# Two fused feed-forward layers: token tiles of 512 columns in place of 480

## The chip, the cores and the metric

One core of one Trainium2 chip. The time is device microseconds of one execution of the program; the median of several runs counts, lower is better.

## What is computed

```python
# x, v: (1, 12480, 128); pos_emb: (12480, 64)
h_filt = (relu(pos_emb @ w1) @ w2) * exp(-0.01 * pos)[:, None]
y = causal convolution of (x * v) with h_filt along the sequence   # by FFT
t = x * y                                  # 12480 tokens x 128
g = relu(t @ w_in) ** 2                    # d_ff 2048
t = g @ w_out
h = t @ w_in2
g = maximum(h, 0) + alpha * minimum(h, 0)
out = g @ w_out2                           # float32 throughout
```

## The kernel before

The long convolution comes first: a small MLP makes the filter, then DFTs as float32 matmuls take the sequence to spectra, multiply them, and take them back. Its last stage is cut into 32 "halves" (16 groups of 4 columns, 2 blocks each, 392 or 388 tokens a half). A half is summed on TensorE (`sum_half`, L742 to L759) and multiplied with the gate x on VectorE into the tensor `x1` (`gate_half`, L761 to L772), which holds all 12,480 tokens as columns on 128 partitions.

The two feed-forward layers (`feed_forward`, L44 to L416) start while the last halves are still to be summed. They work on token tiles of T = 480 columns: NT = 26 tiles. Each layer has F = 2048 hidden features in 16 chunks of 128, taken as PAIRS = 8 pairs. Every product is made from fp32r matmuls on split operands: `hi` (the value rounded to fp32r by a cast on ScalarE) and `lo` (what is left, a subtraction on VectorE). Each product of a chunk is three matmuls, hi x hi, lo x hi, hi x lo: `first_product` (L156 to L158: weights times the tile's x, into the PSUM banks of `h`) and `second_product` (L171 to L173: weights times the activated g, accumulated in a bank of `acc` over all 16 chunks). The weights are loaded anew for each matmul. A PSUM bank has 512 float32 columns, and all PSUM tensors are sliced to `:T`.

Per pair of layer 1: relu on ScalarE (L283, both chunks at once, 960 elements), a square on VectorE (L377) or for the steps in ACT_SQUARES on ScalarE (L287, three pairs of eight), g_hi (ScalarE, L300), g_lo (VectorE, L392). Per pair of layer 2: two signed copies out of PSUM (ScalarE, L311, one chunk each), two leaky activations (VectorE, L351), g_hi (ScalarE, L274), g_lo (VectorE, L363). Per tile: x_hi and x_lo of layer 1 (L258, L338), of layer 2 (L263, L343), and the copy of the result over `x1` (L294), from where SyncE stores it (L136).

The order is written out by hand, for each engine the same. `one_round(i)` has 16 half-steps in which layer 1 works on tile i and layer 2 on tile i-1; a second product comes LAG = 3 half-steps after its first product, so that the ScalarE and VectorE work between the two has time:

```python
for s in range(STEPS):
    if s % 2:      # second product of layer 1, first product of layer 2
        ...
    else:          # first product of layer 1, second product of layer 2
        ...
    for m in late_halves(i, s, 0):
        sum_half(pe, m)
```

`round_0` (L209) weaves tile 0's layer 1 with the first 16 halves. Rounds 1 to STATIC = 8 are unrolled and take two halves each (`late_halves`). Then a hardware loop runs the rounds up to NT - 2 (`full_rounds`, L102), the round NT - 1 is unrolled again, and `drain` (L225) does what is left: layer 2 of the last tile. There the first products alternate between the banks of h[0] and h[1] (`h2_of`). `split_x1(i)` waits until enough halves are gated for the tile's columns (`halves_for`). SyncE's program loads the groups of the convolution's last stage and stores result tiles between them (L133 to L149).

Of the kernel before, what the change touches and what calls it, by code (L numbers as in the profile page):

```python
# [16 lines left out]
T = 480  # L17
# [26 lines left out]
def feed_forward(nc, ctx, mem, x1, ps, last_stage, w_out2, out_t):  # L44
# [7 lines left out]
    NT = S // T  # L52
    PAIRS = F // (2 * P)
    assert NT * T == S and PAIRS == 8
    STEPS = 2 * PAIRS
    LAG = 3
# [76 lines left out]
    def sync_program(sp):  # L133
        def store_out(i):
            sp.wait_ge(out_ready, i + 1)
            sp.dma_start(out_t[:, bass.ds(i * T, T)], x1[:, bass.ds(i * T, T)]).then_inc(out_stored, 16)  # L136

# [9 lines left out]
        with sp.Fori(GROUPS - 11, NT) as i:  # L147
            store_out(i)
        sp.wait_ge(out_stored, 16 * NT)  # L149

    def tensor_program(pe):
        def first_product(layer, pair, into, half_done=None):
            k = 2 * layer
            for c in range(2):
                at = slice((2 * pair + c) * P, (2 * pair + c + 1) * P)
                nc.tensor.matmul(into[:, c, :T], w_hi[k][:, at], x_hi[layer][:], start=True, stop=False)  # L156
                nc.tensor.matmul(into[:, c, :T], w_lo[k][:, at], x_hi[layer][:], start=False, stop=False)  # L157
                last = nc.tensor.matmul(into[:, c, :T], w_hi[k][:, at], x_lo[layer][:], start=False, stop=True)  # L158
# [4 lines left out]
        def second_product(layer, pair, chunk_ready=None):  # L163
            k = 2 * layer + 1
            hi, lo = g_hi[layer][:, pair % 2], g_lo[layer][:, pair % 2]
            for c in range(2):
# [4 lines left out]
                nc.tensor.matmul(acc[layer][:, :T], w_hi[k][:, at], hi[:, c], start=first, stop=False)  # L171
                nc.tensor.matmul(acc[layer][:, :T], w_lo[k][:, at], hi[:, c], start=False, stop=False)  # L172
                last = nc.tensor.matmul(acc[layer][:, :T], w_hi[k][:, at], lo[:, c], start=False, stop=end)  # L173
            return last

        def one_round(i):
            for s in range(STEPS):
                if s % 2:
                    l1, l2 = l1_pair(i, s - LAG), l2_pair(i, s)
                    if within(l1):  # L180
# [3 lines left out]
                        second_product(0, (s - LAG) // 2 % PAIRS).then_inc(g1_used, 1)  # L184
                    if within(l2):
# [5 lines left out]
                        first_product(1, (s - 3) // 2 % PAIRS, h[1], h2_ready).then_inc(h2_ready, 1)  # L191
                else:
                    l1, l2 = l1_pair(i, s), l2_pair(i, s - LAG)
                    if within(l1):
# [3 lines left out]
                        first_product(0, s // 2, h[0]).then_inc(h1_ready, 1)  # L198
                    if within(l2):
# [5 lines left out]
                        second_product(1, (s - LAG - 3) // 2 % PAIRS).then_inc(g2_used, 1)  # L205
# [3 lines left out]
        def round_0():  # L209
            for m in range(ROUND_0):  # L210
                sum_half(pe, m)
                second, first = m - 6, (m - 3) // 2 if m <= 5 else m - 4
                if 0 <= second < PAIRS - 1:
# [3 lines left out]
                    second_product(0, second).then_inc(g1_used, 1)  # L217
                if 0 <= first < PAIRS and m != 4:
# [4 lines left out]
                    first_product(0, first, h[0]).then_inc(h1_ready, 1)  # L223

        def drain():  # L225
            def second(pair):
                pe.wait_ge(g2_lo_ready, pair + 1)
                second_product(1, pair % PAIRS).then_inc(g2_used, 1)
# [19 lines left out]
            second_product(1, PAIRS - 1, last_lo_ready).then_inc(g2_used, 1)  # L248
# [5 lines left out]
    def scalar_program(act):  # L254
        def split_x1(i):
            if isinstance(i, int):
                act.wait_ge(gated, halves_for(S, min((i + 1) * T, S)) if i <= STATIC else HALVES)
            nc.scalar.copy(x_hi[0][:], x1[:, bass.ds(i * T, T)]).then_inc(x1_hi_ready, 1)  # L258

        def split_x2(i):  # L260
            act.wait_ge(g1_used, PAIRS * i)
            wait(act, h2_ready, 2 * PAIRS * (i - 1))
            nc.scalar.copy(x_hi[1][:], acc[0][:, :T]).then_inc(x2_hi_ready, 1)  # L263

        def split_g2(l2, at):
            if isinstance(l2, int) and l2 == PAIRS * NT - 1:
                for c in range(2):
                    act.wait_ge(g2_ready, 2 * l2 + c + 1)
                    wait(act, g2_used, l2 - 1)
                    nc.scalar.copy(g_hi[1][:, at, c], g2[at][:, c]).then_inc(last_hi_ready, 1)  # L270
            else:
                act.wait_ge(g2_ready, 2 * l2 + 2)
                wait(act, g2_used, l2 - 1)
                nc.scalar.copy(g_hi[1][:, at], g2[at]).then_inc(g2_hi_ready, 1)  # L274

        def one_round(i):
            for s in range(STEPS):
                if s % 2 == 0:
                    l1, l2 = l1_pair(i, s), l2_pair(i, s - 1)
                    if within(l1):  # L280
                        act.wait_ge(h1_ready, l1 + 1)
                        wait(act, g1_ready, l1)
                        nc.scalar.activation(relu1[:], h[0][:, :, :T], ACT.Relu).then_inc(relu1_ready, 1)  # L283
                        if s in ACT_SQUARES:
                            act.wait_ge(relu1_ready, l1 + 1)
                            wait(act, g1_lo_ready, l1)
                            nc.scalar.activation(g1[:], relu1[:], ACT.Square).then_inc(g1_ready, 1)  # L287
# [4 lines left out]
                    if s == 4 and (not isinstance(i, int) or i >= 2):  # L292
                        act.wait_ge(g2_used, PAIRS * (i - 1))
                        nc.scalar.copy(x1[:, bass.ds((i - 2) * T, T)], acc[1][:, :T]).then_inc(out_ready, 1)  # L294
                else:
                    l1, l2 = l1_pair(i, s - 1), l2_pair(i, s)
                    if within(l1):
                        act.wait_ge(g1_ready, l1 + 1)
                        wait(act, g1_used, l1 - 1)
                        nc.scalar.copy(g_hi[0][:, s // 2 % 2], g1[:]).then_inc(g1_hi_ready, 1)  # L300
# [34 lines left out]
    def vector_program(dve):  # L335
        def split_x1(i):
            dve.wait_ge(x1_hi_ready, i + 1)
            nc.vector.tensor_tensor(x_lo[0][:], x1[:, bass.ds(i * T, T)], x_hi[0][:].bitcast(FP32),  # L338
                                    ALU.subtract).then_inc(x1_lo_ready, 1)

        def split_x2(i):
            dve.wait_ge(x2_hi_ready, i)
            nc.vector.tensor_tensor(x_lo[1][:], acc[0][:, :T], x_hi[1][:].bitcast(FP32),  # L343
                                    ALU.subtract).then_inc(x2_lo_ready, 1)

        def activate_g2(l2, pair):
# [708 lines left out]
```

## Time and profile before

| | |
|---|---|
| three runs, median | 1435.31 us (1435.1 to 1436.33) |
| the profiled execution | 1434.64 us |
| its span, first to last instruction | 1432.8 us |
| TensorE busy | 1421.2 us, 99% |
| ScalarE busy | 1132.3 us, 79% |
| VectorE busy | 1111.6 us, 78% |
| TensorE clock granted | 1.000 |

Matmuls overlap in the pipe: a record of 0.38 us is longer than the distance to the next start, so the busy times of lines add up to more than the engine's. The pace is read from the distances between starts. A float32 matmul appears as two records, an fp32r matmul as one.

### The profile page before, as it was taken

What the parts mean: (1) busy time and instruction counts of PE and PEld (TensorE: products, weight loads), DVE (VectorE), ACT (ScalarE), POOL (GpSimd) and SP (SyncE); (2) the same over time, 40 slices, a digit from 0 to 9 for tenths busy, and PEclk for the clock granted to TensorE, in tenths of its full rate; (3) what the DMA queues carried; (4) which work ended last, traced back from release to release, by engine and by line L of the source; (5) the groups of instructions that cost most, each with busy time, mean ns of one, the idle gap of its engine ahead of it and who ended that gap; (6) DMA issues with size and microseconds to landing.
All of it is one profiled execution on the core that took longest, in us unless ns stands there. A gap on an engine that the chain in (4) does not pass through costs nothing.

```text
span 1432.8 us, 20481 instructions
## 1 busy us (share of the span) xinstructions
PE 1421.2 (99%) x7002; PEld 1242.0 (87%) x7002; DVE 1111.6 (78%) x1389; ACT 1132.3 (79%) x1553; POOL 70.2 (5%) x61
## 2 busy tenths in 40 slices
PE   8999999999999999999999999999999999999998
PEld 8998888898888888888888888888888888888886
DVE  6876666556877788777888878888887888888787
ACT  3676677556887788777888888888888888888886
POOL 4510011211000000000000000000000000000000
PEclk9999999999999999999999999999999999999999
DMA  8545978442011101100000000000000000000000
GB/s 261 179 145 169 301 222 278 144 142 68 1 30 30 30 0 31 30 8 8 8 7 7 0 7 7 7 7 7 7 0 7 7 7 7 7 7 0 7 8 14
DMA packets 47040, 79.16 MB, mean 55 GB/s; under 512 B 4723, under 2 KB 29529, under 8 KB 46217
## 3 DMA queue, kind: packets, MB, share of 16 engines
q1 hardware_dynamic: 44649, 68.43, 15.2%
q10 hardware_dynamic: 2208, 9.99, 2.0%
q8 instruction: 33, 0.54, 0.2%
q14 instruction: 22, 0.18, 0.0%
q0 software_dynamic: 128, 0.02, 0.0%
HBM read 59.12 MB, written 19.23 MB: 55 GB/s over the span
## 4 chain that ended last, share of the span: by engine, by line
PE 97%; ACT 1%; DVE 1%; issue 0%; DMA 0%; ACTq 0%
PE ps L157 13%; PE ps L171 13%; PE ps L173 13%; PE ps L172 12%; PE ps L158 12%; PE ps L156 12%; PE ps L681 6%; PE ps L647 4%; PE ps L662 3%; PE ps L670 3%; PE ps L758 3%; PE ps L655 1%; PE ps L630 1%; PE ps L725 1%; DVE g_lo L363 0%
## 5 line engine op out<-in xcount | busy, mean ns | idle before, releaser
L363 DVE TENSOR_TENSOR g_lo<-stage,g_hi 128x960 fp32r<-128x960 f32 x207 | 239.5, 1157 | 171.8 <-ACT g_hi L274 171.6
L171 PE MATMUL ps<-g_hi,w_hi 128*128 128x480 f32 x832 | 317.9, 382 | 3.6 <-DVE g_lo L363 2.3
L157 PE MATMUL ps<-x_hi,w_lo 128*128 128x480 f32 x832 | 317.8, 382 | 0.0
L173 PE MATMUL ps<-g_lo,w_hi 128*128 128x480 f32 x832 | 317.4, 381 | 0.0
L172 PE MATMUL ps<-g_hi,w_lo 128*128 128x480 f32 x832 | 316.0, 380 | 0.0
L156 PE MATMUL ps<-x_hi,w_hi 128*128 128x480 f32 x832 | 315.0, 379 | 0.4 <-DVE x_lo L343 0.3
L158 PE MATMUL ps<-x_lo,w_hi 128*128 128x480 f32 x832 | 313.9, 377 | 0.0
L283 ACT ACTIVATE relu<-ps 128x960 f32<-128x960 f32 x208 | 202.8, 975 | 121.5 <-PE ps L158 121.5
L351 DVE SCALAR_TENSOR_TENSOR stage<-stage,alpha_sb 128x480 f32<-128x480 f32 x416 | 279.2, 713 | 3.2 <-ACT stage L311 3.1
L311 ACT ACTIVATE stage<-ps,sign_sb 128x480 f32<-128x480 f32 x416 | 255.1, 656 | 7.6 <-PE ps L158 4.8
L392 DVE TENSOR_TENSOR g_lo<-g,g_hi 128x960 fp32r<-128x960 f32 x208 | 240.8, 1158 | 14.5 <-ACT g_hi L300 14.4
L274 ACT CAST g_hi<-stage 128x960 fp32r<-128x960 f32 x207 | 205.1, 991 | 32.6 <-DVE stage L351 31.3
L300 ACT CAST g_hi<-g 128x960 fp32r<-128x960 f32 x208 | 207.2, 996 | 21.1 <-DVE g L377 17.5
L171 PEld LDWEIGHTS ps<-g_hi,w_hi 128*128 128x128 f32 x832 | 156.1, 188 | 31.4 <-DVE g_lo L363 2.3
L156 PEld LDWEIGHTS ps<-x_hi,w_hi 128*128 128x128 f32 x832 | 156.2, 188 | 29.2 <-issue 2.8
L173 PEld LDWEIGHTS ps<-g_lo,w_hi 128*128 128x128 f32 x832 | 156.2, 188 | 25.2
L172 PEld LDWEIGHTS ps<-g_hi,w_lo 128*128 128x128 f32 x832 | 156.2, 188 | 25.2
L157 PEld LDWEIGHTS ps<-x_hi,w_lo 128*128 128x128 f32 x832 | 156.1, 188 | 23.4
L158 PEld LDWEIGHTS ps<-x_lo,w_hi 128*128 128x128 f32 x832 | 156.2, 188 | 21.6
L377 DVE TENSOR_TENSOR g<-relu 128x960 f32<-128x960 f32 x130 | 150.7, 1159 | 11.6 <-ACT relu L283 11.4
L874 DVE TENSOR_TENSOR work<-ps,work 128x512 f32<-128x512 f32 x98 | 63.2, 687 | 60.4 <-PE ps L662 60.3
L681 PE MATMUL ps<-work 128*128 128x256 f32 x392 | 92.6, 379 | 0.0
(59 smaller groups left out, 1169.2 us busy)
## 6 DMA issues: line engine op xcount, KB each, us to landing
work<-dft_back SPq DMA_DIRECT2D x49, 256.0 KB, 3.2
g_dram<-work SPq DMA_DIRECT2D x49, 256.0 KB, 3.4
gt<-g_dram SPq DMA_DIRECT2D x12, 784.0 KB
gt<-x_seq SPq DMA_DIRECT2D x32, 196.0 KB
work<-v_seq SPq DMA_DIRECT2D x32, 196.0 KB
work<-dft_forward SPq DMA_DIRECT2D x49, 128.0 KB, 3.3
x<-x_gate ACTq DMA_DIRECT2D x4, 1560.0 KB, 8.0
out_t<-x SPq DMA_DIRECT2D x26, 240.0 KB, 2.0
```

Source lines behind the costliest of these rows:

```text
L156: nc.tensor.matmul(into[:, c, :T], w_hi[k][:, at], x_hi[layer][:], start=True, stop=False)
L157: nc.tensor.matmul(into[:, c, :T], w_lo[k][:, at], x_hi[layer][:], start=False, stop=False)
L158: last = nc.tensor.matmul(into[:, c, :T], w_hi[k][:, at], x_lo[layer][:], start=False, stop=True)
L171: nc.tensor.matmul(acc[layer][:, :T], w_hi[k][:, at], hi[:, c], start=first, stop=False)
L172: nc.tensor.matmul(acc[layer][:, :T], w_lo[k][:, at], hi[:, c], start=False, stop=False)
L173: last = nc.tensor.matmul(acc[layer][:, :T], w_hi[k][:, at], lo[:, c], start=False, stop=end)
L274: nc.scalar.copy(g_hi[1][:, at], g2[at]).then_inc(g2_hi_ready, 1)
L300: nc.scalar.copy(g_hi[0][:, s // 2 % 2], g1[:]).then_inc(g1_hi_ready, 1)
L311: nc.scalar.activation(signed_h2[:, c], h2_of(l2)[:, c, :T], ACT.Copy, scale=sign_sb[:, at:at + 1]).then_inc(signed_h2_ready, 1)
L351: nc.vector.scalar_tensor_tensor(out=g2[pair % 2][:, c], in0=signed_h2[:, c], scalar=alpha_sb[:, at:at + 1], in1=signed_h2[:, c], op0=ALU. ...
L363: nc.vector.tensor_tensor(g_lo[1][:, at], g2[at], g_hi[1][:, at].bitcast(FP32), ALU.subtract).then_inc(g2_lo_ready, 1)
L392: nc.vector.tensor_tensor(g_lo[0][:, s // 2 % 2], g1[:], g_hi[0][:, s // 2 % 2].bitcast(FP32), ALU.subtract).then_inc(g1_lo_ready, 1)
```

## The change

Tile 0 has 448 columns, tiles 1 to 23 have 512 and tile 24 has 256: 25 tiles. `width(i)` and `tokens(i)` give a tile's width and its columns in `x1`; with the loop's register as i, the width is T. All buffers that were T wide are 512 wide now, and each instruction is sliced to its tile's width; in a round, layer 1 uses `width(i)` and layer 2 `width(i - 1)`, through `pair_width`. The loop ends one round earlier, and the round NT - 2 is unrolled after it, so that tile NT - 1 meets fixed indices only. The store of the last tile stands behind SyncE's loop. The order of the instructions within a round and in the drain is unchanged.

```diff
-T = 480
+T, EDGE = 512, (448, 256)
...
-    NT = S // T
+    NT = (S - sum(EDGE)) // T + 2
...
+    def width(i):
+        return {0: EDGE[0], NT - 1: EDGE[1]}.get(i, T) if isinstance(i, int) else T
+    def tokens(i):
+        return bass.ds(0 if isinstance(i, int) and i == 0 else i * T - (T - EDGE[0]), width(i))
+    def pair_width(pair):
+        return width(pair // PAIRS) if isinstance(pair, int) else T
...
-        with engine.Fori(STATIC + 1, NT - 1) as i:
+        with engine.Fori(STATIC + 1, NT - 2) as i:
             one_round(i)
+        one_round(NT - 2)
         one_round(NT - 1)
...
-            sp.dma_start(out_t[:, bass.ds(i * T, T)], x1[:, bass.ds(i * T, T)]).then_inc(out_stored, 16)
+            sp.dma_start(out_t[:, tokens(i)], x1[:, tokens(i)]).then_inc(out_stored, 16)
...
-        with sp.Fori(GROUPS - 11, NT) as i:
+        with sp.Fori(GROUPS - 11, NT - 1) as i:
             store_out(i)
+        store_out(NT - 1)
...
-                nc.tensor.matmul(into[:, c, :T], w_hi[k][:, at], x_hi[layer][:], start=True, stop=False)
+                nc.tensor.matmul(into[:, c, :t], w_hi[k][:, at], x_hi[layer][:, :t], start=True, stop=False)
...
-            hi, lo = g_hi[layer][:, pair % 2], g_lo[layer][:, pair % 2]
+            hi, lo = g_hi[layer][:, pair % 2, :, :t], g_lo[layer][:, pair % 2, :, :t]
...
-                nc.tensor.matmul(acc[layer][:, :T], w_hi[k][:, at], hi[:, c], start=first, stop=False)
+                nc.tensor.matmul(acc[layer][:, :t], w_hi[k][:, at], hi[:, c], start=first, stop=False)
...
-                act.wait_ge(gated, halves_for(S, min((i + 1) * T, S)) if i <= STATIC else HALVES)
-            nc.scalar.copy(x_hi[0][:], x1[:, bass.ds(i * T, T)]).then_inc(x1_hi_ready, 1)
+                act.wait_ge(gated, halves_for(S, sum(map(width, range(i + 1)))) if i <= STATIC else HALVES)
+            nc.scalar.copy(x_hi[0][:, :width(i)], x1[:, tokens(i)]).then_inc(x1_hi_ready, 1)
...
-                        nc.scalar.activation(relu1[:], h[0][:, :, :T], ACT.Relu).then_inc(relu1_ready, 1)
+                        nc.scalar.activation(relu1[:, :, :width(i)], h[0][:, :, :width(i)], ACT.Relu).then_inc(relu1_ready, 1)
...
-                nc.vector.tensor_tensor(g_lo[1][:, at], g2[at], g_hi[1][:, at].bitcast(FP32),
-                                        ALU.subtract).then_inc(g2_lo_ready, 1)
+                nc.vector.tensor_tensor(g_lo[1][:, at, :, :t], g2[at][:, :, :t],
+                                        g_hi[1][:, at, :, :t].bitcast(FP32), ALU.subtract).then_inc(g2_lo_ready, 1)
```

The other matmuls, casts, activations and subtractions of the two layers are sliced in the same way.

## Rows read from the trace of the kernel before

**Rows 1.** The page, part 1: busy us (share of the span) and instructions

```profile
PE 1421.2 (99%) x7002; PEld 1242.0 (87%) x7002; DVE 1111.6 (78%) x1389; ACT 1132.3 (79%) x1553; POOL 70.2 (5%) x61
```

**Rows 2.** The page, part 4: the chain that ended last, by line

```profile
PE ps L157 13%; PE ps L171 13%; PE ps L173 13%; PE ps L172 12%; PE ps L158 12%; PE ps L156 12%; PE ps L681 6%; PE ps L647 4%; PE ps L662 3%; PE ps L670 3%; PE ps L758 3%; PE ps L655 1%; PE ps L630 1%; PE ps L725 1%; DVE g_lo L363 0%
```

**Rows 3.** Busy time in two stretches, columns in the first line

```profile
core 0: us, PE busy (x) PEld busy (x) DVE busy (x) ACT busy (x) POOL busy (x), PEclk, DMA share, GB/s
727.76:1354.70 626.94, 626.94 (x2882) 539.31 (x2881) 518.16 (x586) 546.91 (x691) 0.00 (x0) 1.00 0.02 6
459.52:685.92 226.40, 226.40 (x1122) 198.03 (x1121) 178.01 (x206) 181.83 (x231) 0.00 (x0) 1.00 0.06 17
```

**Rows 4.** Line L338, x_lo of layer 1: 26 tiles

```profile
L338 DVE TENSOR_TENSOR x_lo<-x,x_hi x26: 647/659/662, 288.1 to 1354.7; 128x480 fp32r<-128x480 f32 x26
```

**Rows 5.** Timeline of PE in a steady round: start, us, line

```profile
902.34 0.38 PE L171 MATMUL ps<-g_hi,w_hi 128*128 128x480 f32 x1
...
902.77 0.39 PE L173 MATMUL ps<-g_lo,w_hi 128*128 128x480 f32 x1
903.00 0.38 PE L171 MATMUL ps<-g_hi,w_hi 128*128 128x480 f32 x1
...
904.96 0.37 PE L156 MATMUL ps<-x_hi,w_hi 128*128 128x480 f32 x1
```

**Rows 6.** The chain in the convolution: start, us, what

```profile
95.53 1.73 PE ps L681 x8
```

**Rows 7.** Groups of instructions: busy us, mean ns, idle before

```profile
L351 DVE SCALAR_TENSOR_TENSOR stage<-stage,alpha_sb 128x480 f32<-128x480 f32 x416 | 279.2, 713 | 3.2 <-ACT stage L311 3.1
...
L363 DVE TENSOR_TENSOR g_lo<-stage,g_hi 128x960 fp32r<-128x960 f32 x207 | 239.5, 1157 | 171.8 <-ACT g_hi L274 171.6
L274 ACT CAST g_hi<-stage 128x960 fp32r<-128x960 f32 x207 | 205.1, 991 | 32.6 <-DVE stage L351 31.3 <-PE ps L173 0.3
...
L359 DVE TENSOR_TENSOR g_lo<-stage,g_hi 128x480 fp32r<-128x480 f32 x2 | 1.3, 658 | 0.0
L270 ACT CAST g_hi<-stage 128x480 fp32r<-128x480 f32 x2 | 1.2, 592 | 0.8 <-DVE stage L351 0.7
```

**Rows 8.** Timeline of VectorE and ScalarE in a steady round

```profile
902.98 1.34 DVE L351 SCALAR_TENSOR_TENSOR stage<-stage,alpha_sb 128x480 f32<-128x480 f32 x2
...
904.36 1.00 ACT L274 CAST g_hi<-stage 128x960 fp32r<-128x960 f32 x1 [0.58 <-DVE stage L351]
...
905.39 1.16 DVE L363 TENSOR_TENSOR g_lo<-stage,g_hi 128x960 fp32r<-128x960 f32 x1
...
906.46 1.15 DVE L392 TENSOR_TENSOR g_lo<-g,g_hi 128x960 fp32r<-128x960 f32 x1
...
907.53 0.71 DVE L351 SCALAR_TENSOR_TENSOR stage<-stage,alpha_sb 128x480 f32<-128x480 f32 x1
```

**Rows 9.** Timeline of PE in the drain: where it waited

```profile
1410.87 0.46 PE L171 MATMUL ps<-g_hi,w_hi 128*128 128x480 f32 x1 [1.62 <-DVE g_lo L363]
...
1416.55 0.49 PE L171 MATMUL ps<-g_hi,w_hi 128*128 128x480 f32 x1 [0.22 <-DVE g_lo L363]
...
1422.26 0.48 PE L171 MATMUL ps<-g_hi,w_hi 128*128 128x480 f32 x1 [0.22 <-DVE g_lo L363]
```

**Rows 10.** Timeline at the drain's beginning, ScalarE and VectorE

```profile
1406.69 0.56 ACT L294 COPY x<-ps 128x480 f32<-128x480 f32 x1 [0.99 <-PE ps L173]
...
1409.57 1.16 DVE L363 TENSOR_TENSOR g_lo<-stage,g_hi 128x960 fp32r<-128x960 f32 x1
```

**Rows 11.** Timeline of the end

```profile
1429.32 0.37 PE L173 MATMUL ps<-g_lo,w_hi 128*128 128x480 f32 x1
1429.73 0.56 ACT L294 COPY x<-ps 128x480 f32<-128x480 f32 x1 [1.72 <-PE ps L173]
```

More of the change, by code:

```diff
@@ L155, in first_product @@
                 at = slice((2 * pair + c) * P, (2 * pair + c + 1) * P)
-                nc.tensor.matmul(into[:, c, :T], w_hi[k][:, at], x_hi[layer][:], start=True, stop=False)
-                nc.tensor.matmul(into[:, c, :T], w_lo[k][:, at], x_hi[layer][:], start=False, stop=False)
-                last = nc.tensor.matmul(into[:, c, :T], w_hi[k][:, at], x_lo[layer][:], start=False, stop=True)
+                nc.tensor.matmul(into[:, c, :t], w_hi[k][:, at], x_hi[layer][:, :t], start=True, stop=False)
+                nc.tensor.matmul(into[:, c, :t], w_lo[k][:, at], x_hi[layer][:, :t], start=False, stop=False)
+                last = nc.tensor.matmul(into[:, c, :t], w_hi[k][:, at], x_lo[layer][:, :t], start=False, stop=True)
                 if c == 0 and half_done is not None:
@@ L216, in round_0 @@
                     pe.wait_ge(g1_lo_ready, second + 1)
-                    second_product(0, second).then_inc(g1_used, 1)
+                    second_product(0, second, width(0)).then_inc(g1_used, 1)
                 if 0 <= first < PAIRS and m != 4:
@@ L222, in round_0 @@
                     wait(pe, relu1_ready, first)
-                    first_product(0, first, h[0]).then_inc(h1_ready, 1)
+                    first_product(0, first, width(0), h[0]).then_inc(h1_ready, 1)
         def drain():
@@ L262, in split_x2 @@
             wait(act, h2_ready, 2 * PAIRS * (i - 1))
-            nc.scalar.copy(x_hi[1][:], acc[0][:, :T]).then_inc(x2_hi_ready, 1)
+            t = width(i - 1)
+            nc.scalar.copy(x_hi[1][:, :t], acc[0][:, :t]).then_inc(x2_hi_ready, 1)
         def split_g2(l2, at):
+            t = pair_width(l2)
             if isinstance(l2, int) and l2 == PAIRS * NT - 1:
@@ L273, in split_g2 @@
                 wait(act, g2_used, l2 - 1)
-                nc.scalar.copy(g_hi[1][:, at], g2[at]).then_inc(g2_hi_ready, 1)
+                nc.scalar.copy(g_hi[1][:, at, :, :t], g2[at][:, :, :t]).then_inc(g2_hi_ready, 1)
         def one_round(i):
@@ L337, in split_x1 @@
             dve.wait_ge(x1_hi_ready, i + 1)
-            nc.vector.tensor_tensor(x_lo[0][:], x1[:, bass.ds(i * T, T)], x_hi[0][:].bitcast(FP32),
+            nc.vector.tensor_tensor(x_lo[0][:, :width(i)], x1[:, tokens(i)], x_hi[0][:, :width(i)].bitcast(FP32),
                                     ALU.subtract).then_inc(x1_lo_ready, 1)
@@ L342, in split_x2 @@
             dve.wait_ge(x2_hi_ready, i)
-            nc.vector.tensor_tensor(x_lo[1][:], acc[0][:, :T], x_hi[1][:].bitcast(FP32),
+            t = width(i - 1)
+            nc.vector.tensor_tensor(x_lo[1][:, :t], acc[0][:, :t], x_hi[1][:, :t].bitcast(FP32),
                                     ALU.subtract).then_inc(x2_lo_ready, 1)
         def activate_g2(l2, pair):
+            t = pair_width(l2)
             wait(dve, g2_lo_ready, l2 - 1)
```

57 lines of the change are left out of this document (31 added, 26 removed).

## The prediction

> **What bounds the kernel now.** I read the busy table first: TensorE is busy for 99% of the span, VectorE 78%, ScalarE 79% [rows 1]. The chain of waits says the same of the path: six matmul lines of the two layers (L156 to L158, L171 to L173) carry 75% of it [rows 2]. Then the stretches. The loop's fifteen rounds between the x_lo of 727.76 and that of 1354.70 take 626.94 us, 41.80 each, with TensorE busy in all of it at clock 1.00; ScalarE has 546.91 (36.5 a round) and VectorE 518.16 (34.5) [rows 3, 4]. The five unrolled rounds from 459.52 take 45.28 each: the same round with two halves of the convolution's last stage, 32 matmul records, so 3.48/32 = 0.109 us per record. TensorE is the bound by 5 us a round. A round has 8 pairs of chunks x 2 layers x 2 products x 6 matmuls = 192 matmuls, so one costs 41.75/192 = 0.2174 us, if 0.05 us is set aside for the longer handoff at its start; the starts in the timeline lie 0.21 to 0.23 apart [rows 5].
>
> **The question is what that 0.2174 is made of.** At 2.4 GHz 480 columns stream in 0.200 us, so 0.0174 is extra. The convolution's float32 passes have almost none: 8 passes of 256 columns in 1.73 us [rows 6] are 0.216 each, which is two cycles a column (0.2133) and 0.003; the 128-column record of 0.109 is 0.1067 and 0.002. Each of these loads 128 columns of weights too. The fp32r matmul streams at twice that rate, and something is lost. It could be lost once per matmul (the weight load that runs beside it), or in proportion to columns. No row has an fp32r matmul of another width, so the split is bounded from the two sides: per matmul all 17.4 ns or none.
>
> **Part A, one round fewer.** 26 tiles become 25: 23 of 512, one of 448, one of 256. The columns stay 12,480 x 192 / 2.4 GHz = 998.4 us. The extra stays 192 x 26 x 0.0174 = 86.9 us if it goes with columns, and falls to 83.5 us if it goes with matmuls: -3.3, and -0.05 for the handoff, -3.4. I take the per-matmul value: the passes at half rate, with the same weight loads, show that the stream alone loses only 2 to 3 ns, and a weight load is of one size whatever the tile. A 512-column matmul is then 0.2307 us, one of 256 0.1241.
>
> The Trainium skill (TensorE: Matmul & The Clock Gate, Back-to-back issue gap) gives columns / 2.4 + 2.5 ns between matmuls. The float32 passes agree with that; the fp32r ones do not (it would be 202.5 ns, the trace has 217.4). What it would make of the change is the second rival.
>
> **Part B, the steady round, ScalarE and VectorE.** Per pair they process columns at the slopes that the one- and two-chunk forms show: the cast goes from 592 to 991 ns over 480 elements (0.83 ns each), the subtraction from 658 to 1157 (1.04) [rows 7]. From 480 to 512 a round gains 2336 elements on ScalarE (+1.9 us, 38.4) and 1920 or so on VectorE (+2.0, 36.5), against a TensorE round of 192 x 0.2307 = 44.3. Cost nothing: TensorE covers them with 6 us. If that cover went (a 512-column matmul at 0.216, a round of 41.5), 3 us would be left. The dependent ring, VectorE's two activations, ScalarE's g_hi, VectorE's g_lo for both layers, comes round in 4.55 us of 5.22 now [rows 8]; at 512 some 4.8 of 5.5.
>
> **Part C, the round before the last.** There layer 1 works on 256 columns while layer 2 has 512. TensorE needs 12 x 0.1241 + 12 x 0.2307 = 4.26 us a pair. The ring: two activations 1.33, handoff 0.12, g_hi 1.05, handoff 0.03, layer 2's g_lo 1.14, layer 1's g_lo on 512 elements 0.60 = 4.27, if the square (0.60) hides beside g_hi; 4.87 if it doesn't. Loss 0 to 8 x 0.61 = 4.9 us. LAG lets three half-steps pass before a product is wanted, so I take 0.5.
>
> **Part D, the drain.** In the last eight pairs only layer 2 runs. Two pairs take 5.7 us (restarts at 1410.87, 1416.55, 1422.26 [rows 9]) for 24 matmuls, 5.22: 0.24 lost a pair. At 256 columns TensorE needs 12 x 0.1241 = 1.49 a pair; VectorE 0.88 for the two activations and 0.69 for g_lo, 1.57; with the same 0.35 of handoffs as now (2.86 less VectorE's 1.34 + 1.16) it is 1.92. Loss per pair 0.08 to 0.43 against 0.24 now: over eight -1.3 to +1.5; with the shorter cover of the first and last pairs I take +1.0, range -1.3 to +2.5. The wait of 1.62 at its beginning stays: from the out copy at 1406.69 to the end of g_lo at 1410.73 is 4.0 us [rows 9, 10] under twelve matmuls of 2.6; after it is about 3.0 under 1.5. The time moved out of the drain is no gain by itself, since those columns are worked elsewhere.
>
> **Part E, the ends.** The last output copy falls from 0.56 to 0.37 us [rows 11] and the last half splits by some tenths under a shorter cover: -0.2 (-0.5 to 0). The first x_hi and x_lo are 32 columns shorter: -0.06. Same two halves of the convolution are needed for 448 columns as for 480 (the first has 392). Later tiles ask for halves that the unrolled rounds produce ahead: at the end of round i the kernel has 16 + 2i halves, 6240 + 780i columns, and wants 448 + 512(i + 1). SP's queue issues one store fewer and the same group loads, now spaced by rounds 3 us longer; none is near a wait. One more round is unrolled and the loop has 14 turns instead of 16: the unrolled and the looped rounds differ by the 32 records alone, so nothing.
>
> **Sum**: -3.4 + 0.5 + 1.0 - 0.2 - 0.1 = -2.2 us against the profiled execution's 1434.64 (span 1432.8 and 1.84 around it): 1432.4. The median of the runs is 0.67 above the profiled one, so 1433.1, or -0.15%. A measurement can tell about 0.2%, 2.9 us. This forecast's own range is 1429 to 1437: A's zero and the ends of C and D.
>
> **Rivals.**
> 1. *The weights' read and the stream share one rate.* 1920 + 512 bytes per partition in 0.2174 us is 11.19 bytes a ns; then 512 columns take 0.2288, 448 0.2059, 256 0.1372: -9.0 instead of -3.4, with the rest -7.8: 1427.5. For it: the half-rate passes, which need less, lose nothing. Against: a weight load's record has the same length in both kinds.
> 2. *The extra goes with columns* and only some 3 ns with the matmul: A gives -0.6; 1435.9. This is what the skill's rule would leave of A too, if the unexplained 15 ns are taken as a slower stream. For it: nothing in these rows excludes it.
> 3. *A floor near 0.216 for any fp32r matmul*, whatever its width up to a bank: the 480-column one lasts as long in its record (0.38) as a float32 pass of 512 cycles. Then a round costs 41.8 as now and one is gone: -41.8 for the round and +1.2 for the rest, 1394.7. Against: spacings of 0.21 are seen [rows 5], under a floor of 0.216.
> 4. *Slower, by the ring* of part C: the square doesn't hide (4.87 a pair, +4.9) and the drain runs at 1.92 a pair (+2.5): 1433.1 + 4.4 + 1.5 = 1439. It decides from a ring of about 4.8 us a pair in that round; below 4.3 it is nothing. For it: ScalarE does three of the eight squares itself, ahead of g_hi. Against: the lag.
> 5. *Slower, by a steeper extra*: starts are up to 0.23 apart now; if every 512-column matmul had an extra of 22 ns, it would be 4416 x 4.6 ns = +20: 1453. It needs only +1.2 ns over my 0.2307 to be measurably slower.
>
> **Chances.** Forecast 0.47 (faster 0.20, same 0.24, slower 0.03); rival 1 0.14, rival 2 0.12 (same 0.10, slower 0.02), rival 3 0.09, rival 4 0.10, rival 5 0.08. Faster 0.43, same 0.34, slower 0.23. The range 1424 to 1441 holds the forecast and rivals 1, 2 and 4, and leaves out rival 3 and most of 5, with a remainder of rival 1's uncertainty.
>
> **What would show it.** The loop's round: 44.3 us (44.0 by rival 1, 44.6 by rival 2, 41.8 by rival 3), that is 0.2307 between matmul starts. Matmuls of 256 columns in the last tile 0.124 apart (0.116 by rival 2, 0.137 by rival 1). PE busy share of 99% still. In the drain L171 waits for g_lo, of 0.1 to 0.5 us per pair; the round before it without waits on L363 or L392 if C is small. A steady round in which TensorE waits for any engine would make the whole prediction wrong.

## The result, and the profile after

The changed kernel takes 1418.93 us (median of four runs, 1418.68 to 1420.0) against 1435.36: a ratio of 0.9886, 95% interval 0.9869 to 0.9903. That is 16.4 us less, where 2.2 were forecast, and below the range that was given. The profiled execution took 1420.0, with a span of 1418.1; in it the convolution ended late, for the first x_lo starts at 289.6 us instead of 288.1.

The busy table and the chain of waits by line, after:

```profile
PE 1405.2 (99%) x6810; PEld 1196.3 (84%) x6810; DVE 1104.5 (78%) x1350; ACT 1124.0 (79%) x1507; POOL 70.2 (5%) x61
```

```profile
PE ps L169 12%; PE ps L184 12%; PE ps L171 12%; PE ps L170 12%; PE ps L186 12%; PE ps L185 12%; PE ps L703 6%; PE ps L669 5%; PE ps L780 3%; PE ps L684 3%; PE ps L692 3%; PE ps L677 1%; PE ps L652 1%; DVE stage L371 1%; DVE g_lo L384 1%
```

TensorE is still busy for 99% of the span, and the chain still runs through the six matmul lines, now L169 to L171 and L184 to L186, at 72% [rows 1, 2]. The bound is the same engine. So the gain is in what TensorE does, or in how fast it does it. Busy time in thirteen looped and five unrolled rounds, with the columns in the first line, and the line that marks the rounds' ends:

```profile
core 0: us, PE busy (x) PEld busy (x) DVE busy (x) ACT busy (x) POOL busy (x), PEclk, DMA share, GB/s
742.82:1310.96 568.14, 568.14 (x2498) 467.55 (x2497) 474.47 (x508) 499.44 (x599) 0.00 (x0) 1.00 0.02 6
463.01:699.11 236.10, 236.10 (x1121) 198.08 (x1120) 187.24 (x206) 191.94 (x231) 0.00 (x0) 1.00 0.06 17
```

```profile
L356 DVE TENSOR_TENSOR x_lo<-x,x_hi x25: 425/691/695, 289.6 to 1354.2; 128x512 fp32r<-128x512 f32 x23, 128x448 fp32r<-128x448 f32 x1, 128x256 fp32r<-128x256 f32 x1
```

A looped round takes 568.14 / 13 = 43.70 us, an unrolled one 236.10 / 5 = 47.22. The forecast for the looped one was 44.3. Per column of the tile it is 85.4 ns against 87.1 before [rows 3]. VectorE has 474.47 / 13 = 36.5 us a round and ScalarE 38.4: both as worked out in part B. The timeline of TensorE in a looped round shows where the rest comes from:

```profile
898.45 0.39 PE L186 MATMUL ps<-g_lo,w_hi 128*128 128x512 f32 x1
898.68 0.39 PE L184 MATMUL ps<-g_hi,w_hi 128*128 128x512 f32 x1
898.90 0.39 PE L185 MATMUL ps<-g_hi,w_lo 128*128 128x512 f32 x1
899.13 0.39 PE L186 MATMUL ps<-g_lo,w_hi 128*128 128x512 f32 x1
899.36 0.39 PE L184 MATMUL ps<-g_hi,w_hi 128*128 128x512 f32 x1
...
900.04 0.39 PE L184 MATMUL ps<-g_hi,w_hi 128*128 128x512 f32 x1
```

Eight starts in a row lie 0.2267 us apart, 1.36 for six matmuls, where before six took 1.30 to 1.31 with distances that went up and down, 0.21 to 0.23 in the two decimals of the view [rows 5]. In the records' nanoseconds nearly all of the changed kernel's distances in the looped rounds are 226 or 227 (2389 of 2495; the others are a few of 228 and seven at each turn of a round, 224 to 332); before they ran 220, 219, 213, 221, 210, 217, and nearly all lay between 210 and 223. The groups of the 512-column forms, busy time, mean ns and idle time before them, grew as forecast:

```profile
L371 DVE SCALAR_TENSOR_TENSOR stage<-stage,alpha_sb 128x512 f32<-128x512 f32 x368 | 259.3, 746 | 0.0
...
L384 DVE TENSOR_TENSOR g_lo<-stage,g_hi 128x1024 fp32r<-128x1024 f32 x184 | 225.2, 1224 | 163.2 <-ACT g_hi L289 163.2
...
L289 ACT CAST g_hi<-stage 128x1024 fp32r<-128x1024 f32 x184 | 192.4, 1046 | 43.0 <-DVE stage L371 32.4 <-PE ps L186 10.6
```

746 ns against 713, 1224 against 1157, 1046 against 991 [rows 7].

The waits of TensorE from the round before the last to the end, in the timeline:

```profile
1365.53 0.50 PE L184 MATMUL ps<-g_hi,w_hi 128*128 128x512 f32 x1 [0.28 <-DVE g_lo L384]
...
1391.15 0.50 PE L184 MATMUL ps<-g_hi,w_hi 128*128 128x512 f32 x1 [0.53 <-DVE g_lo L384]
...
1395.42 0.50 PE L184 MATMUL ps<-g_hi,w_hi 128*128 128x512 f32 x1 [0.55 <-DVE g_lo L384]
...
1399.09 0.50 PE L184 MATMUL ps<-g_hi,w_hi 128*128 128x512 f32 x1 [1.03 <-DVE g_lo L384]
...
1403.50 0.36 PE L184 MATMUL ps<-g_hi,w_hi 128*128 128x256 f32 x1 [1.31 <-DVE g_lo L384]
...
1407.04 0.39 PE L184 MATMUL ps<-g_hi,w_hi 128*128 128x256 f32 x1 [0.42 <-DVE g_lo L384]
...
1410.60 0.39 PE L184 MATMUL ps<-g_hi,w_hi 128*128 128x256 f32 x1 [0.36 <-DVE g_lo L384]
...
1412.48 0.39 PE L184 MATMUL ps<-g_hi,w_hi 128*128 128x256 f32 x1 [0.19 <-DVE g_lo L384]
...
1414.55 0.39 PE L184 MATMUL ps<-g_hi,w_hi 128*128 128x256 f32 x1 [0.32 <-DVE g_lo L380]
```

Before there were fewer of them [rows 9]. The loss can be counted as the time between starts beyond the pace (0.2174 us before; 0.2268 and 0.1188 now), which takes in that a matmul after a wait lasts some 0.1 us longer. Over the last round and the drain it is 8.7 us against 4.9 before: 2.0 against nothing in the last 192 matmuls ahead of the drain, 6.7 against 4.8 in the drain, which begins at 1391.15. (The 6.8 and 4.9 of the expectations below are about those of the drain alone.) Of the 2.0, the wait before 1391.15 has 0.7, and 0.4 is no wait at all: the 512-column matmuls are slower there. Six of them, between groups of 256 columns:

```profile
1360.89 0.40 PE L184 MATMUL ps<-g_hi,w_hi 128*128 128x512 f32 x1
...
1362.28 0.28 PE L184 MATMUL ps<-g_hi,w_hi 128*128 128x256 f32 x1
```

That is 1.39 us for six, not 1.36. In the two rounds of this kernel where groups of 512 columns stand between groups of 448 or of 256, and nobody waits, their distances average 231 ns.

In the drain proper two pairs take 3.54 and 3.56 us (1403.50, 1407.04, 1410.60), 1.78 a pair, between the 1.57 and 1.92 of part D. The end:

```profile
1415.29 0.28 PE L186 MATMUL ps<-g_lo,w_hi 128*128 128x256 f32 x1
1415.60 0.37 ACT L310 COPY x<-ps 128x256 f32<-128x256 f32 x1 [1.17 <-PE ps L186]
```

From the last matmul's start to the end of the span it is 2.8 us, 3.5 before [rows 11].

### The profile page after: what moved, and what is told of

The parts are those of the page before. It is cut to its first block, busy times and chain, and to the rows that moved or that the text cites. A ratio compares the mean times of both kernels' runs of the same rounds, so it can differ in the third digit from the quotient of the medians.

```text
span 1418.1 us, 19798 instructions
## 1 busy us (share of the span) xinstructions
PE 1405.2 (99%) x6810; PEld 1196.3 (84%) x6810; DVE 1104.5 (78%) x1350; ACT 1124.0 (79%) x1507; POOL 70.2 (5%) x61
## 4 chain that ended last, share of the span: by engine, by line
PE 94%; DVE 3%; ACT 1%; issue 1%; DMA 0%; ACTq 0%; DVEq 0%
PE ps L169 12%; PE ps L184 12%; PE ps L171 12%; PE ps L170 12%; PE ps L186 12%; PE ps L185 12%; PE ps L703 6%; PE ps L669 5%; PE ps L780 3%; PE ps L684 3%; PE ps L692 3%; PE ps L677 1%; PE ps L652 1%; DVE stage L371 1%; DVE g_lo L384 1%
## 5 line engine op out<-in xcount | busy, mean ns | idle before, releaser
L384 DVE TENSOR_TENSOR g_lo<-stage,g_hi 128x1024 fp32r<-128x1024 f32 (+2 forms) x199 | 238.7, 1200 | 169.1 <-ACT g_hi L289 169.0
L184 PE MATMUL ps<-g_hi,w_hi 128*128 128x512 f32 (+2 forms) x800 | 309.7, 387 | 5.9 <-DVE g_lo L384 4.7
L169 PE MATMUL ps<-x_hi,w_hi 128*128 128x512 f32 (+2 forms) x800 | 310.6, 388 | 0.1
L171 PE MATMUL ps<-x_lo,w_hi 128*128 128x512 f32 (+2 forms) x800 | 307.4, 384 | 0.0
L186 PE MATMUL ps<-g_lo,w_hi 128*128 128x512 f32 (+2 forms) x800 | 307.2, 384 | 0.0
L170 PE MATMUL ps<-x_hi,w_lo 128*128 128x512 f32 (+2 forms) x800 | 307.2, 384 | 0.0
L185 PE MATMUL ps<-g_hi,w_lo 128*128 128x512 f32 (+2 forms) x800 | 307.2, 384 | 0.0
L371 DVE SCALAR_TENSOR_TENSOR stage<-stage,alpha_sb 128x512 f32<-128x512 f32 (+2 forms) x400 | 276.5, 733 | 3.7 <-ACT stage L329 3.6
L329 ACT ACTIVATE stage<-ps,sign_sb 128x512 f32<-128x512 f32 (+2 forms) x400 | 251.2, 673 | 3.5 <-PE ps L171 2.0
L415 DVE TENSOR_TENSOR g_lo<-g,g_hi 128x1024 fp32r<-128x1024 f32 (+2 forms) x200 | 239.7, 1198 | 14.0 <-ACT g_hi L317 13.7
L184 PEld LDWEIGHTS ps<-g_hi,w_hi 128*128 128x128 f32 x800 | 150.2, 188 | 37.2 <-DVE g_lo L384 5.0
L169 PEld LDWEIGHTS ps<-x_hi,w_hi 128*128 128x128 f32 x800 | 150.3, 188 | 33.9 <-issue 4.2
L171 PEld LDWEIGHTS ps<-x_lo,w_hi 128*128 128x128 f32 x800 | 150.3, 188 | 29.8
L186 PEld LDWEIGHTS ps<-g_lo,w_hi 128*128 128x128 f32 x800 | 150.2, 188 | 29.7
```

What stands on the lines that cost most here:

```text
L169: nc.tensor.matmul(into[:, c, :t], w_hi[k][:, at], x_hi[layer][:, :t], start=True, stop=False)
L170: nc.tensor.matmul(into[:, c, :t], w_lo[k][:, at], x_hi[layer][:, :t], start=False, stop=False)
L171: last = nc.tensor.matmul(into[:, c, :t], w_hi[k][:, at], x_lo[layer][:, :t], start=False, stop=True)
L184: nc.tensor.matmul(acc[layer][:, :t], w_hi[k][:, at], hi[:, c], start=first, stop=False)
L185: nc.tensor.matmul(acc[layer][:, :t], w_lo[k][:, at], hi[:, c], start=False, stop=False)
L186: last = nc.tensor.matmul(acc[layer][:, :t], w_hi[k][:, at], lo[:, c], start=False, stop=end)
```

## The experiments

In all of them the whole reference is computed. "Distance" is the time from a matmul's start to the next one's in the records, averaged without the places where TensorE waited or a round turned. "A looped round" is the mean of thirteen, between starts of the x_lo subtraction. In the looped rounds of all these kernels TensorE waits for no other engine. e2, p1, p2, q1, q2 and the five of s were run once each, for their traces; their times have no interval.

**The theories.** After the result the size of one 512-column matmul was the whole question: 0.2267 us where the forecast had 0.2307. Theory 1: the pace is a matter of the number of columns. Theory 2: it is a matter of where the operand tiles lie in SBUF, for 512 columns of four bytes are 2048 bytes, and with them every x and g tile starts at the same place modulo 2048.

**e1: 480 columns in tiles 512 apart.**

```diff
-T, EDGE = 512, (448, 256)
+T, EDGE = 480, (480, 480)
+BW = 512
...
-        late = {"x1_hi": (T,), "x1_lo": (T,), "relu1": (2, T), ...
+        late = {"x1_hi": (BW,), "x1_lo": (BW,), "relu1": (2, BW), ...
```

> Tiles of 480 columns as before (26 tiles), but the operand tiles in SBUF lie 512 columns apart, as in the change; nothing else differs from the kernel before except that round NT - 2 is unrolled. In the changed kernel a 512-column fp32r matmul follows the one before it after 0.2267 us in the loop, where 0.2307 was forecast. Theory 1, the pace depends on the number of columns alone: here 0.2174 us between starts, a loop round of 41.8 us, and 1435 us. Theory 2, the pace depends on where the operand tiles start (multiples of 2048 bytes): here 0.200 + 0.0134 = 0.2133 us, a round of 41.0, and 1435.3 - 20 = 1415 us.

```profile
727.80:1269.80 542.00, 542.00 (x2498) 467.01 (x2497) 448.99 (x507) 473.46 (x599) 0.00 (x0) 1.00 0.02 6
```

A round of 41.69 us and a distance of 216.75 ns (217.42 before); 1432.69 us, ratio to before 0.9979 (0.9970 to 0.9989). Theory 2 as it stood, with 0.2133 for 480 columns, is wrong. But the pace did move a little with the place alone.

**e5: 512 columns in tiles 528 apart.**

```diff
+BW = 528
...
-        late = {"x1_hi": (T,), "x1_lo": (T,), "relu1": (2, T), ...
+        late = {"x1_hi": (BW,), "x1_lo": (BW,), "relu1": (2, BW), ...
```

> The changed kernel with its operand tiles 528 columns (2112 bytes) apart in SBUF. Theory 1, columns alone: 0.2267 us between starts, a loop round of 43.7 us and 1418.9 us, no change. Theory 2, addresses: the forecast 0.2307 us, a round of 44.5 and 1418.9 + 18 = 1437 us.

```profile
749.27:1328.19 578.92, 578.92 (x2498) 468.60 (x2497) 474.66 (x508) 501.87 (x599) 0.00 (x0) 1.00 0.02 6
```

A round of 44.53 us, a distance of 231.9 ns, and 1438.05 us: 19 us slower than the changed kernel by nothing but the gaps between tiles, and slower than the kernel before (1.0015, 1.0006 to 1.0025). This is the forecast's matmul, 0.2307 with 1 ns more. Theory 1 alone falls: with 512 columns the place decides 5 ns of each matmul. That the number of columns counts beside the place is seen in e1, where 480 columns at the change's places keep an extra of 16.8 ns.

**e2: eleven other widths in one kernel.**

```diff
-T, EDGE = 512, (448, 256)
+T, FIRST = 512, (448, 480, 504, 384, 496, 320, 192, 508, 464)
...
-        for i in range(1, STATIC + 1):
+        for i in range(1, UNROLL + 1):        # UNROLL = 10
```

> Tiles 0 to 8 of 448, 480, 504, 384, 496, 320, 192, 508 and 464 columns, then 16 of 512 and one of 492: one profile gives the distance between matmul starts at each width. Known: 256 columns 0.1188 (12.1 ns over the stream at 2.4 GHz), 448 0.2026 (15.9), 480 0.2174 (17.4), 512 0.2267 (13.3). Theory 1a, a cost per matmul plus a cost per column on a smooth curve, 512 being the exception: 504 and 508 at 0.2285 and 0.230, above 512. Theory 1b, the extra falls gradually above 480: 496 at 0.222, 504 at 0.2245, 508 at 0.226. At 320 and 384 both say 13 to 15 ns over the stream (0.1467, 0.1745). A rule with a threshold at 256 columns would put 192 far above 0.092; without one it is 0.092, or the 0.109 at which the float32 passes go, if the weight load bounds it.

1430.05 us in one run. (The rest of the edit gives tiles 0 to 8 their own widths.) The timeline, first matmul of six of that width and the one after the six, for 384, 496, 192, 508 and 464 columns:

```profile
465.52 0.34 PE L177 MATMUL ps<-x_hi,w_hi 128*128 128x384 f32 x1
...
466.56 0.38 PE L177 MATMUL ps<-x_hi,w_hi 128*128 128x496 f32 x1
...
521.03 0.39 PE L177 MATMUL ps<-x_hi,w_hi 128*128 128x496 f32 x1
...
522.37 0.31 PE L177 MATMUL ps<-x_hi,w_hi 128*128 128x320 f32 x1
...
582.36 0.25 PE L177 MATMUL ps<-x_hi,w_hi 128*128 128x192 f32 x1
582.45 0.27 PE L178 MATMUL ps<-x_hi,w_lo 128*128 128x192 f32 x1
...
583.00 0.42 PE L177 MATMUL ps<-x_hi,w_hi 128*128 128x508 f32 x1
...
615.90 0.39 PE L177 MATMUL ps<-x_hi,w_hi 128*128 128x508 f32 x1
...
617.26 0.38 PE L177 MATMUL ps<-x_hi,w_hi 128*128 128x464 f32 x1
...
661.14 0.37 PE L177 MATMUL ps<-x_hi,w_hi 128*128 128x464 f32 x1
...
662.40 0.39 PE L177 MATMUL ps<-x_hi,w_hi 128*128 128x512 f32 x1
```

| columns | 192 | 256 | 320 | 384 | 448 | 464 | 480 | 492 | 496 | 504 | 508 | 512 |
|---|---|---|---|---|---|---|---|---|---|---|---|---|
| distance, ns | 111.6 | 118.8 | 146.0 | 174.5 | 204.5 | 209.6 | 216.8 | 221.2 | 223.6 | 228.0 | 228.5 | 226.8 |
| over columns / 2.4 GHz | 31.6 | 12.1 | 12.7 | 14.5 | 17.8 | 16.3 | 16.8 | 16.2 | 16.9 | 18.0 | 16.8 | 13.5 |

(256 is from the changed kernel.) Tiles lie 512 columns apart here for every width. Up to 508 the extra grows slowly, from 12 ns at 256 columns to 16 to 18 near 500: part of it goes with the matmul, part with the columns. At 512 it is 13.5.

The single values hold to some 4 ns only, for all widths but 512 have one tile here, whose matmuls stand between those of two other widths, and the neighbours count. The same 448 columns at the same places have 202.7 between groups of 512 in the changed kernel and 206.4 between groups of 480 here. 508 columns have 228 between groups of 464 and 229.6 between groups of 512 (two groups only); and the 512-column matmuls between groups of 508 (two again) have 230.3, where those between groups of 464 or 492 keep 226.6. So the table does not show that 512 columns start sooner after each other than 508 would in rounds of their own; against the 480 columns of e1, which have such rounds, the smaller extra of 512 is shown. At 192 columns the distance is 109 to 117 ns inside a group, 32 over the stream, but 85 to 93 from the first matmul after a wider group (582.36 to 582.45), so a floor is not shown.

**e4: 496 columns.**

```diff
-T, EDGE = 512, (448, 256)
+T, EDGE = 496, (320, 256)
```

> 24 tiles of 496 columns, one of 320 first and one of 256 last (26 tiles). If the extra per matmul is that of 480 columns (17.4 ns) a 496-column matmul takes 0.2241 and the whole time is that of before, less some 1 us at the ends: 1434 to 1436. If the gain comes gradually with width, 0.222 and 24 x 192 x 2.1 ns less: 1425. A loop round is 43.1 or 42.7 us.

```profile
726.55:1286.84 560.29, 560.29 (x2497) 467.90 (x2496) 461.64 (x508) 487.26 (x599) 0.00 (x0) 1.00 0.02 6
```

A round of 43.10 us, a distance of 224.4; 1437.71 us, 1.0017 (1.0008 to 1.0027). The extra is 17.7 ns, that of 480 columns, so the gain does not come gradually with width. (Tiles are 1984 bytes apart here, so this is not the place of the change either.) The time was above what was expected by 2 us: this kernel has as many tiles as before and the narrow last tile's waits (4.5 us on g_lo, as the changed kernel's 4.7) without anything that pays for them.

**p1 and p2: which tiles have to be alike.** In the first the sets are shifted against their weights, each as a whole; in the second the tiles of one set against each other.

```diff
# p1_phase; elements of 4 bytes
+        pads = {"g1_hi": 16, "x2_hi": 24, "g2_hi": 32, "w3_hi": 56}
         for n, shape in late.items():
+            if n in pads:
+                sb(f"pad_{n}", [P, pads[n]])
# p2_strides
+        pads = {"x1_lo": 16, "relu1": 112, "g1_lo": 16, "x2_hi": 112, "g2_lo": 448, "w3_hi": 64}
-                "g2_hi": (2, 2, T), "g2_lo": (2, 2, T),
+                "g2_hi": (2, 2, T + 16), "g2_lo": (2, 2, T + 16),
```

> The changed kernel, all operand tiles still 512 columns apart within a product's set, but each set shifted against the weights: layer 1's x by 0, layer 1's g by 64 bytes, layer 2's x by 160, layer 2's g by 288 (the weights of the last product stay put). If what counts is that the starts of the moving tiles are alike modulo 2048 bytes, whatever the weights' own, all four products keep 0.2267 us between starts inside each group of six. If it is the place of the moving tile against that of the weights, each set has another pace, between 0.216 (no extra) and 0.231.

> The changed kernel with x_lo of layer 1 moved 64 bytes against x_hi, g_lo of layer 1 moved 64 bytes against g_hi, layer 2's x as in the change, and layer 2's g with its chunks 528 columns apart instead of 512. If successive moving tiles must start alike, layer 2's first product stays at 0.2267 and the three others rise towards 0.231; if only the distance between chunks mattered, layer 2's second product alone would rise.

Both are at 1436.5 us, in one run each. Distances in p1, by set: layer 1's x (not shifted) 228.4, and inside it 226.6 to 226.9 in its last four matmuls of six; layer 1's g (64 bytes) 228.8; layer 2's x (160) 234.8; layer 2's g (288) 233.7. In each of these sets hi, lo and both chunks start alike, so alike starts within a set are not enough. In p2 all four lie between 230.4 and 232.4, layer 2's untouched x too (230.4), against the forecast. The reading that fits is that a set loses the fast pace when its neighbours on TensorE have lost it, as the 512-column groups between 448 or 256 columns do in the changed kernel. (In p1 the last set's weights moved by 512 bytes; modulo 256 its shift of 288 is one of 32.)

**r: everything together by 32 bytes.**

```diff
+        pads = {"x1_hi": 8}
```

> The changed kernel with all operand tiles moved together by 32 bytes, the fourth set of weights (w_out2) with them: layer 1's x and g and layer 2's x are shifted against their weights by 32 bytes, layer 2's g is not, and all moving tiles still start alike modulo 2048. Theory 1, moving tiles must start alike: all four sets stay at 0.2267 us and the time at 1418.9. Theory 2, the place against the weights counts: three sets at about 0.234 as the two sets shifted by 160 and 288 bytes had, layer 2's g at 0.2267 except where it follows a shifted set; 3300 x 7 ns = 23 us more, 1442.

```profile
751.18:1331.84 580.66, 580.66 (x2498) 467.96 (x2497) 474.69 (x508) 502.08 (x599) 0.00 (x0) 1.00 0.02 6
```

A round of 44.67 us and 1441.3 us, 1.0039 (1.0025 to 1.0054): slower by 22 us than the changed kernel, whose program it is, with 32 bytes of nothing ahead of the tiles. All moving tiles start alike, and yet the three sets shifted against their weights have 233.8, 233.3 and 233.0. The fourth, whose weights moved with it, has 230.4: faster than they, not 226.7. The forecast of theory 2 came in for the time and the three sets; for the fourth only if its neighbours disturb it throughout, for its distances swing between 224 and 235 inside the six.

**q1 and q2: other shifts, set by set.**

```diff
# q1_phase
+        pads = {"x1_hi": 32, "g1_hi": 16, "x2_hi": 84, "g2_hi": 4, "w3_hi": 120}
# q2_phase
+        pads = {"x1_hi": 16, "g1_hi": 16, "x2_hi": 32, "g2_hi": 32, "w3_hi": 32}
```

> As p1_phase, with shifts against the weights of 128 bytes (layer 1's x), 192 (layer 1's g), 16 (layer 2's x) and 32 (layer 2's g). If the grain is 64 bytes, the first two stay at 0.227 to 0.229 and the last two are at 0.233 to 0.235. If the pace fell smoothly away from a best place, 16 and 32 bytes would be the nearest to 0.2267 and 128 and 192 the worst.

> As p1_phase, with shifts of 64 bytes (layer 1's x), 128 (layer 1's g), 256 (layer 2's x) and 384 (layer 2's g). With a grain of 64 bytes all four lie at 0.2267 to 0.229 and the time near 1419 to 1424; a pace below 0.225 in one of them would show a better place than the change's.

1438.54 and 1437.56 us. All eight sets lie between 230.6 and 233.0, whatever their shift: 16, 32, 64, 128, 192, 256 and 384 bytes. Neither expectation held. If each of four sets at four places disturbs the next, as p2 suggests, such a kernel cannot tell the rule; uniform shifts can.

**s: uniform shifts of 64, 128, 256, 512 and 2048 bytes.**

```diff
+        pads = {"x1_hi": 16}     # s_shift64; 32, 64, 128 and 512 in the others
```

> All operand tiles moved together by 64 bytes. If only a 64-byte grain counts: 0.2267 us between starts and 1419. If the place within a larger block counts: 0.229 to 0.234 and 1430 to 1442.

> All operand tiles moved together by 256 bytes. 0.2267 us and 1419 if the place counts modulo 256 bytes or less; 0.229 to 0.234 and 1430 to 1442 otherwise.

> All operand tiles moved together by 512 bytes, the length of one chunk of weights, so that the distance to the weights is the same modulo 512. If the place against the weights counts, 0.2267 us and 1419; if the absolute place modulo 2048 counts, 0.229 to 0.234 and 1430 to 1442.

> All operand tiles moved together by 2048 bytes. By every theory of places modulo 2048 or less this is the changed kernel: 0.2267 us and 1419. If it is not, the place has nothing to do with the pace in this simple way.

> All operand tiles moved together by 128 bytes (w_out2's split with them). The uniform shifts so far: 64 bytes put the three sets whose distance to their weights changed at 0.229 and left the fourth at 0.2268; 256, 512 and 2048 bytes change nothing. If the distance to the weights counts modulo 128 bytes, this is 0.2267 us and 1419; if modulo 256, three sets lie near 0.229 to 0.231 and the fourth at 0.2267, 1425 to 1433.

Thirteen looped rounds of s_shift64:

```profile
744.71:1316.11 571.40, 571.40 (x2498) 467.69 (x2497) 474.25 (x508) 499.10 (x599) 0.00 (x0) 1.00 0.02 6
```

of s_shift128:

```profile
749.21:1328.50 579.29, 579.29 (x2497) 469.67 (x2496) 474.60 (x508) 502.13 (x599) 0.00 (x0) 1.00 0.02 6
```

of s_shift256:

```profile
742.31:1310.41 568.10, 568.10 (x2498) 467.45 (x2497) 474.33 (x508) 499.52 (x599) 0.00 (x0) 1.00 0.02 6
```

| shift, bytes | time, us | a looped round | the three sets, ns | the fourth, ns |
|---|---|---|---|---|
| 0 (the change) | 1418.93 | 43.70 | 226.7 to 227.1 | 226.8 |
| 32 | 1441.3 | 44.67 | 233.0 to 233.8 | 230.4 |
| 64 | 1425.31 | 43.95 | 228.9 to 229.2 | 226.8 |
| 128 | 1438.88 | 44.56 | 232.6 to 233.3 | 229.5 |
| 256 | 1419.44 | 43.70 | 226.7 to 227.1 | 226.7 |
| 512 | 1419.21 | 43.70 | 226.7 to 227.1 | 226.7 |
| 2048 | 1419.38 | 43.71 | 226.7 to 227.1 | 226.8 |

The three sets' distance to their weights changed by the shift, the fourth's did not. 256 bytes and its multiples change nothing; 32, 64 and 128 cost 1.6%, 0.4% and 1.4%. The times at 64 and 128 bytes lie outside both ranges that were expected for each. At 64 bytes the split is clean: the fourth set keeps its pace, the three others lose 2.2 ns. So the place of the moving tile against its weights, modulo 256 bytes, counts, and theory 2 stands in this form: among groups of its own width, a 512-column matmul has the pace of 0.2267 where all tiles have one place modulo 256 bytes against their weights. It is not the whole rule: at 32 and 128 bytes the fourth set loses 3 ns too. That may be the neighbours again; that the fourth set's own place in SBUF, or its weights', counts as well was not excluded, for no run moved weights and tiles of all four sets together.

**e3, e6 and e7: other edges.**

```diff
-T, EDGE = 512, (448, 256)
+T, EDGE = 512, (256, 448)      # e3_swap; (512, 192) in e6, (320, 384) in e7
```

> Edges exchanged: 256 columns first, 448 last. The matmuls are the same in number and width. The changed kernel's TensorE waits after 1360 us add up to 6.8 us, with 480 columns in both last rounds they were 4.9 (before); theory: the narrow last tile costs some 1.9 us of waits and saves 0.2 at the last copy, so this gives 1418.9 - 1.7 = 1417.2 us. Rival: the narrow last tile shortens the end, and this is 1 to 2 us slower, 1420.5.

> 24 tiles of 512 and a last one of 192. The columns are the same; the pace of 192 columns was 0.1116 us, so a set of 25 matmuls takes 24 x 0.2267 + 0.1116 = 5.552 us against 5.536 in the change: +3.2 us over 192 sets. With the drain bound by VectorE, 8 x 0.2 us less than at 256 columns at best, or as much more: 1420.5 to 1423.5.

> Edges of 320 and 384 columns: 0.1460 + 0.1745 against 0.2026 + 0.1188 us a set, -0.9 ns x 192 = -0.2 us. The waits at the end lie between the change's 6.8 us and the 5.2 with 448 last; the waits in the first two rounds, which 256 columns first raised by some 2 us, between too. So 1418.9 - 0.2 and within 1 us: 1417.7 to 1419.2. If the two kinds of wait each fall off faster than in proportion, this is the best of the three splits by 1 us, and no more.

1419.68 us (0.9889, 0.9873 to 0.9906), 1421.26 (0.9900, 0.9884 to 0.9917) and 1418.49 (0.9883, 0.9867 to 0.9899). e6 and e7 came out as expected; e3 is 2.5 us above its forecast and 0.8 below its rival's. TensorE's waits for g_lo near the end, for the change, e3 and e7:

```profile
PE ps L184 <- DVE g_lo L384: 4.7, 8, 1.3
```

```profile
PE ps L184 <- DVE g_lo L384: 2.8, 5, 1.6
```

```profile
PE ps L184 <- DVE g_lo L384: 3.1, 5, 1.4
```

With 448 columns last the waits there fall by 1.9 us as expected. But the time does not: 256 columns first leave TensorE waiting in the first two rounds, 0.4 us for the relu (the first products come too close), 0.4 for a transfer into gt, and on g_lo and x_lo 0.6, 0.7 and 0.3: 2.4 us in waits where the change has 1.0. What one end gives the other takes. The middle split is 0.4 us below the change, less than the intervals can tell.

## Why the prediction was wrong

**The step that failed is part A**, and in it one term, the time of a 512-column matmul. It had 0.2307 us, all of the 17.4 ns of extra per matmul; measured are 0.2267 in the looped rounds, an extra of 13.3, below both of its bounds. Without the lucky places it would have been near: e4's 17.7 ns at 496 columns is the extra of 480 (17.4), and e5, 512 columns in tiles 528 apart, has a distance of 231.9. The split itself was too simple: the 12.1 ns at 256 columns lie between the 17.4 of "all per matmul" and the 9.3 of "all per column". What the prediction held for certain was that the extra depends on nothing but these two. Both bounds were drawn from rows in which only an average of 17.4 was read, and the distances between 0.21 and 0.23 [rows 5] were averaged, when they were the sign of something: with weight loads and matmuls all of one size the extra went from 10 to 23 ns. That it depends on how the reads of weights and tile meet, and that with tiles of 2048 bytes they meet in the same way each time, is the reading that fits the shifts; it is argued, not shown.

The bill, before against after: 4992 x 0.2174 = 1085.3 us of matmuls; 4416 x 0.2271 + 192 x 0.2026 + 192 x 0.1188 = 1064.6: -20.7 where -3.3 stood. (0.2271 takes in the slower groups beside the narrow tiles.) Of what part A missed, the 512-column matmuls have 15.9 us, those of 256 columns 1.0 and those of 448 0.3. Against it stands the time beyond the pace: +1.7 at the turns and in the first rounds, +3.5 in the last round and the drain (parts C and D, forecast +1.5; it is the 8.7 against 4.9 of above without the slower groups, which 0.2271 has already); the ends give -0.8 (forecast -0.3). The sum is -16.3, and from the first x_lo to the end the profiled executions differ by -16.2. The turn of a looped round costs 43.70 - 192 x 0.2268 = 0.16 us, not the 0.05 set aside. It shows only where 512-column matmuls are fast: some 0.09 us in s_shift64, while in e5, r_shift32 and s_shift128 no distance of the looped rounds is above 241 ns, so nothing is lost there. Why it grew was not tried.

**Point by point.** Part B held to a tenth: 38.4 and 36.5 us of the two engines in a round of 43.7. Part C: the last round before the drain lost 2.0 us where 0.5 was forecast, 0.4 of it by the slower 512-column groups. Its pairs take 4.26 to 4.28 us, not the 4.87 of rival 4's ring. Part D: +1.9 where +1.0 was forecast, inside its range. The pairs at 1.78 us are as worked out; the beginning is not "what it was", for four waits of 0.5, 0.6, 1.0 and 1.3 us stand there in place of 1.6 and three short ones. Part E: the last copy takes 0.37 us, to the letter, and what follows it is 0.4 us shorter too. The unrolled round cost nothing: e1, with that and the spacing, is no slower than before.

**The rivals.** Rival 1, one rate for both reads, came nearest in time (1427.5) and was wrong in its sizes: it had 0.2059 and 0.1372 us at 448 and 256 columns, measured 0.2026 and 0.1188. Rival 2 is half true in e2, and no part of the gain. Rival 3's floor does not exist: 448 columns go at 0.2026 and 256 at 0.1188. Rival 5 named what e5 and r_shift32 have, a steeper extra, if a smaller one than its 22 ns: 1438 and 1441 us, not 1453. It was an accident of the buffers' places in this program that decided between it and the result, and no row of before could show it.

The Trainium skill (TensorE: Matmul & The Clock Gate, Step-by-step: what each phase is for) says that loading the next weights takes no SBUF read bandwidth from the running matmul. For the float32 passes the rows fit (3 ns over the stream). For fp32r the runs speak against it: moving the tiles by 32 bytes against the weights costs 6 to 7 ns of 227. That the two reads meet in the memory is the reading that fits; the runs show that places count, not the circuit behind it.

**What stays open.** Why 256 bytes; why 512 columns have the even pace and the small extra, and 480 columns at the same places (e1, 216.8) do not; why groups of 512 lose it beside groups of 448, 256 or 508 columns and keep it beside 464 and 492; and whether any place gives 512 columns an extra below 13.3 ns: none of the places tried did.

## What to carry to other kernels

An fp32r matmul of 512 columns whose weights are loaded anew each time costs 0.2267 or up to 0.235 us by nothing but the places of its tiles in SBUF: lay moving tiles out 2048 bytes apart (2112 cost 5 ns a matmul), all at the same distance to the weights modulo 256 bytes, keep narrower matmuls out of their neighbourhood, and look at the distances between starts, for even ones are the sign of it. Before an unexplained part of an instruction's time is carried over to a new size, ask whether its single values scatter, and widen the range by that scatter. A narrow tile at either end moves waits about rather than saving them: three splits of the same 704 columns lie within 1.2 us, and the one that ends on 192 is 2.3 us above the change.

## What was not expected of the hardware

- 512 columns: a distance of 226.67 ns, which at 2.4 GHz is 544 cycles, among groups of their own width; between groups of 448 or 256 columns it is 231.
- 32 bytes of padding ahead of the operand tiles: +22 us, 1418.9 to 1441.3, in a program otherwise the same.
- fp32r matmuls of 256 columns 118.8 ns apart and of 192 columns 111.6: no jump up below 256 columns, and little gain.
